# First sort of a two-layer MoE kernel in two parts: one between the scan's later chunks, one beside layer 0

## What is computed

```python
# scan: x, f_logit (2, 5056, 256)
f = lower_bound + (1 - lower_bound) * sigmoid(f_logit)
h[t] = f[t] * h[t-1] + (1 - f[t]) * x[t]
# layer 0 (x = h, 10112 rows)
xn = x / (norm(x) + 1e-6);  en = emb / (norm(emb) + 1e-6)
logits = xn @ en.T / tau
# layer 1 (x = output of layer 0)
logits = x @ w_gate
# both
e = argmax(logits); p = softmax(logits)[e]      # sum + 1e-9
out[row] = p * (relu(x[row] @ w1[e]) @ w2[e])
```

## Time and profile before

| | |
|---|---|
| time, median of 3 runs | 1383.54 us (1382.56 to 1385.02) |
| time of the profiled execution | 1383.36 us |
| its span, first to last instruction | 1381.6 us |
| TensorE busy in the span | 1329.6 us |
| VectorE, ScalarE, GpSimd busy | 971.5, 835.2, 439.2 us |
| mean granted clock | 0.973 |

### The profile page before, as it was taken

One profiled execution on the slowest core, in us unless ns is written; L12 is line 12 of the kernel. 1 busy time (PEld: TensorE's weight loads), 2 busy tenths in 40 slices (PEclk: granted clock), 3 DMA queues, 4 the chain that ended last, 5 costly groups with the idle time before them and its releaser, 6 DMA issues.

```text
span 1381.6 us, 31343 instructions
## 1 busy us (share of the span) xinstructions
PE 1329.6 (96%) x11005; PEld 1299.6 (94%) x11005; DVE 971.5 (70%) x1468; ACT 835.2 (60%) x1402; POOL 439.2 (32%) x458
## 2 busy tenths in 40 slices
PE   7994799999999999999999999999999999999996
PEld 6993399999999999999999999899999999999996
DVE  5878476666666666669876679777777777777773
ACT  4774166666666666666656566556666666666663
POOL 4663221121221211222111234323444444444431
PEclk9995599999999999999999999999999999999999
DMA  8983686666665656668856668546666666666650
GB/s 256 329 275 104 64 273 193 213 199 194 203 198 200 199 195 214 198 193 154 254 166 192 209 202 217 174 153 212 221 217 213 226 226 216 221 213 219 222 186 1
DMA packets 204662, 276.83 MB, mean 200 GB/s; under 512 B 33350, under 2 KB 171988, under 8 KB 204596
## 3 DMA queue, kind: packets, MB, share of 16 engines
q1 hardware_dynamic: 191060, 240.74, 56.7%
q0 software_dynamic: 13536, 35.21, 7.6%
HBM read 242.69 MB, written 35.18 MB: 201 GB/s over the span
## 4 chain that ended last, share of the span: by engine, by line
PE 91%; DVE 4%; issue 1%; ACT 1%; POOL 1%; DMA 1%; SPq 0%; ACTq 0%; DVEq 0%; POOLq 0%
PE bank L1306 39%; PE bank L1324 38%; PE bank L1240 4%; PE bank L1290 3%; PE bank L1335 2%; PE bank L1344 1%; PE bank L1203 1%; PE bank L1222 1%; PE bank L1216 1%; DVE hT L381 1%; DVE gx L371 1%; POOL fg L888 1%; ACT sq L1063 0%; DMA fin<-in_f_logit 0%; ACT th L1049 0%
## 5 line engine op out<-in xcount | busy, mean ns | idle before, releaser
L1306 PE MATMUL bank<-xs,w1h 128*128 128x256 f32 x3008 | 570.5, 288 | 1.5 <-DVE xs L656 1.5
L1119 ACT ACTIVATE hh<-bank 128x512 fp32r<-128x512 f32 x376 | 225.2, 599 | 413.6 <-PE bank L1306 413.6
L1306 PEld LDWEIGHTS bank<-xs,w1h 128*128 128x128 f32 x3008 | 461.5, 189 | 3.2 <-DVE xs L656 1.9
L667 DVE SCALAR_TENSOR_TENSOR hl<-bank,hh 128x512 fp32r<-128x512 f32 x376 | 259.9, 691 | 249.3 <-ACT hh L1119 246.9
L1324 PE MATMUL bank<-w2h,hl 128*128 128x256 f32 x1504 | 423.1, 281 | 0.0
L1324 PE MATMUL bank<-w2l,hh 128*128 128x256 f32 x1504 | 422.5, 281 | 0.0
L1324 PE MATMUL bank<-w2h,hh 128*128 128x256 f32 x1504 | 421.7, 280 | 0.0
L1306 PE MATMUL bank<-xs,w1l 128*128 128x256 f32 x1504 | 421.6, 280 | 0.0
L1306 PEld LDWEIGHTS bank<-xs,w1l 128*128 128x128 f32 x1504 | 283.7, 189 | 0.0
L1324 PEld LDWEIGHTS bank<-w2h,hh 128*128 128x128 f32 x1504 | 283.3, 188 | 0.0
L1324 PEld LDWEIGHTS bank<-w2l,hh 128*128 128x128 f32 x1504 | 283.1, 188 | 0.0
(11 more groups left out here) (160 smaller groups left out, 1039.6 us busy)
## 6 DMA issues: line engine op xcount, KB each, us to landing
w1raw<-in_moe_w SPq DMA_DIRECT2D x94, 1024.0 KB
w2raw<-in_moe_w SPq DMA_DIRECT2D x94, 1024.0 KB, 5.6
rows_b<-yb SPq DMA_DIRECT2D x94, 128.0 KB, 2.3
xin<-in_x SPq DMA_DIRECT2D x19, 512.0 KB, 6.0
fin<-in_f_logit SPq DMA_DIRECT2D x19, 512.0 KB, 7.9
rows_a<-h_rows SPq DMA_DIRECT2D x19, 512.0 KB, 5.6
xb<-rows_a,row_i POOLq DMA_INDIRECT x94, 4.9
xb<-rows_b,row_i POOLq DMA_INDIRECT x94, 4.9
```

Source lines behind the costliest of these rows:

```text
L667: v.scalar_tensor_tensor(hl[:, j, :], bank[j % UB][:, :], 0.0, hh[:, j, :].bitcast(fp32), ALU.max, ALU.subtract).then_inc(hid_lo, 1)
L1119: nc.scalar.activation(hh[:, j, :], bank[j % UB][:, :], ACT.Relu).then_inc(hid_hi, 1)
L1306: ins = mm(bank[j % UB][:, f * GW:(f + 1) * GW], w[:, p, o:o + P], xs[:, p, a, c * GW:(c + 1) * GW], start=k == 0, stop=k == 3 * DC - 1)
```

## The change

- The first sort has two parts, as layer 1's has. `PARTS` lists all four: (0, 40 tiles), (all 79), (0, 64), (all 94). The first part sorts the tokens of chunks 0 to 9 into 12 whole pairs, with 24 slot tiles; the second sorts those left over with the other tokens into 35 pairs, with 70 slot tiles.
- Part 0 runs in ticks between the scan's chunks 11 to 19, three in each, on every engine (`beside_scan`). Part 1 runs in ticks beside layer 0's pairs from pair 0 on. The first 12 pairs gather from the first 5120 rows of `rows_a`.
- SyncE loads the weights of pairs 0 and 1 in those ticks, after it has waited for the experts, and then stores the first pair list (5120 items). The second is stored beside layer 0.
- The chunks from 11 on are written out, not looped.
- Since the second part needs whole chunks in time order, a chunk is loaded with four consecutive tokens on a partition (4 KB in one piece), and the transposes of the load write to PSUM with a step of four, so that time runs along a row as before.
- GpSimd writes its tables of numbers ahead of the scan, and its norms follow the rows by two chunks instead of three.
- Counting takes `EXPERTS_AT_ONCE` = 4, 2, 4, 2 experts with both counts in one PSUM bank.
- In layer 0 the transposes of y stand at one place of a step for both tiles (two steps after the pair), its logits a step later (`old`), each kept with one copy. Layer 1's sorts start later by half a pair and one pair.
- Weights' second buffers share memory with the scan's buffers. VectorE waits for the scan's last stores before the first hidden result.
- For layer 1's second part the waits for the pair list and the stored rows stand behind a gather, beside the wait for the slots.

```diff
+    K1 = 10
+    T1 = K1 * CH
+    P1 = (T1 * P - E * (GW - 1)) // GW
...
+        PARTS = [(0, T1, T1, G * P1, 0, P1), (T1, TT, TT, ST - G * P1, P1, NP - P1),
+                 (0, TA, TA, G * PA, 0, PA), (TA, ST, ST, ST - G * PA, PA, NP - PA)]
+        FRONT = [20, 21, 22, 21]
+        OH_AT = [2, 2, 4, 2]
+        EXPERTS_AT_ONCE = [4, 2, 4, 2]
...
+        def beside(parts):
+
+            def tick(i):
+                if i.var is None and i.const >= NP + 3:
+                    next(parts[3], None)
+                elif i.var is None and i.const >= XA + 3:
+                    next(parts[2], None)
+                elif i.var is None and i.const < XA:
+                    next(parts[1], None)
             return tick
 
-        FRONT = [18, 15]
+        def beside_scan(part):
+            def tick(k):
+                if k.var is None and k.const > K1:
+                    next(part, None)
+            return tick
...
@@ VectorE, scan step
                     v.tensor_tensor_scan(hT[:, c, par, 0:w], fg[:, c, 0:w], gx[:, c, 0:w],
                                          hT[:, c, 1 - par, CW - 1:CW], ALU.mult,
                                          ALU.subtract).then_inc(h_ok, 1)
+                    tick(i)
                 if i.var is not None or i.const > 0:
                     keep_logits(i.plus(-1), CH)
+                tick(i)
...
@@ VectorE, after the scan
+            keep_logits(Index(NCH - 1), tiles_in(NCH - 1))
+            for c in range(DC):
+                split_w1_lo(Index(0), c)
+            finish(parts[0])
+            for half in range(2):
+                split_w2_lo(Index(0), half)
...
@@ SyncE
+            def sort(q):
+
+                lo, hi = PARTS[q][0:2]
+                for _ in range(OH_AT[q] + 2 * len(groups(q)) + 6):
+                    yield
+                if q == 0:
+                    sp.wait_ge(dve_c, mark["experts", q])
+                    for i in (Index(0), Index(1)):
+                        read_expert(i)
+                        load_w1(i)
+                        load_w2(i)
+                        yield
+                sp.wait_ge(dve_c, mark["pair", q])
+                sp.dma_start((rows_av if q < 2 else rows_bv)[:, lo:hi, D:D + 2], pair[:, lo:hi, :]
+                             ).then_inc(pair_out, 16)
...
@@ TensorE
                     for dst, src in ((bank[c], xin), (bank[2 + c], fin)):
+                        in_time = dst[:, 0:nt * P].rearrange("p (q j) -> p q j", j=nt)
                         for j in range(nt):
-                            ins = nc.tensor.transpose(dst[:, j * P:(j + 1) * P],
+                            ins = nc.tensor.transpose(in_time[:, :, j],
                                                       src[:, sx, j * D + c * P:j * D + (c + 1) * P],
                                                       ident[:, :])
...
             def a_step(i):
                 a_front(i, CH if i.var is not None else tiles_in(i.const))
+                tick(i)
+                tick(i)
                 if i.var is not None or i.const > 0:
                     a_back(i.plus(-1), CH)
+                tick(i)
...
+                for b, e, k, number in groups(q):
+                    if b == 0:
+                        pe.wait_ge(dve_c, mark["oh", q])
+                    else:
+                        pe.wait_ge(dve_c, mark["counted", q, b - 1])
+                    mm(sum_of(q, T), ones_b[:, :], oh[:, e:e + k, 0:T], start=True, stop=True)
+                    mm(cum_of(q, T), upto[:, :], oh[:, e:e + k, 0:T], start=True, stop=True).then_inc(pe_s, 1)
+                    yield
+                    yield
...
+            pe.wait_ge(tanh_ok, 2 * NCH)
+            pe.wait_ge(g_ok, 2 * NCH)
+            pe.wait_ge(rows_ok, NCH)
+            pe.wait_ge(lg_kept, NCH)
+            pe.wait_ge(dve_c, mark["slots", 0])
             turn_x(Index(0))
...
@@ TensorE, one pair
                 if here(i) and here(nxt):
                     turn_x(nxt)
+                if here(old) and layer_of(old) == 0:
+                    y_logits(old)
                 if here(last2) and layer_of(last2) == 0:
-                    y_logits(last2, 1)
-                tick(i, 1)
+                    turn_y(last2)
+                tick(i)
...
@@ GpSimd, one pair
+                if i.var is None and i.const == P1 - 3:
+                    pool.wait_ge(dve_c, mark["slots", 1])
+                    pool.wait_ge(pair_out, 32)
+                    for b in range(2):
+                        pool.wait_ge(h_out[b], 16 * ((NCH + 1 - b) // 2))
+                if i.var is None and i.const == NP - 3:
+                    pool.wait_ge(dve_c, mark["slots", 2])
+                if i.var is None and i.const == NP + PA - 3:
+                    pool.wait_ge(dve_c, mark["slots", 3])
+                    pool.wait_ge(pair_out, 64)
                     for s in range(2 * G):
                         pool.wait_ge(y_out[s], stored(s, NP))
```

More of the change, by code:

```diff
@@ L1278, in resort @@
                     yield
-                    if q % 3 == 2:
+                    if q >= 2 and c % 3 == 2:
                         yield
+            parts = [sort(q) for q in range(2 * LY)]
+            tick = beside_scan(parts[0])
+            run_steps(pe, 0, K1 + 1, a_step, LOOP_K, 0)
+            for k in range(K1 + 1, NCH):
+                a_step(Index(k))
+            a_back(Index(NCH - 1), tiles_in(NCH - 1))
+            finish(parts[0])
+            tick = beside(parts)
             def turn_x(i):
```

702 lines of the change are left out of this document (311 added, 391 removed).

## The result

| | before | after |
|---|---|---|
| time, median | 1383.81 us (1382.56 to 1385.02, 20 runs) | 1388.91 us (1383.08 to 1393.68, 20 runs) |
| ratio after / before | | 1.0034, 95% interval 1.0022 to 1.0047 |
| profiled execution, its span | 1383.36, 1381.6 us | 1386.24, 1384.5 us |

The change makes the kernel 5.1 us slower; the forecast was 4.5 us faster. The time lies in the range that was given, the sign is wrong. By the profiled executions the difference is 2.9 us; where the other 2 us are is told with the last of the experiments.

A forecast was written before the change was run, and what follows sets the result against it. TensorE was taken to bound the pairs, one serial sort the gap after the scan. Terms: -42.0 + 22.0 + 21.0 + 0.3 - 5.8 = -4.5 us, forecast 1379.0 us, range 1368 to 1397.

The forecast's parts named there:

- What bounds the kernel: Kernel before: pairs are paid in TensorE time only; between scan and pairs it waits 60.4 us for one serial sort.
- The scan grows: Chunks 11 to 19 carry the first sort: VectorE becomes the bound, a loss of 22 us, bounds 14.4 and 41.
- Rival 3: Scan: lighter TensorE work brings the lower clock for half the stretch; growth 33 in place of 22, 1390 us; chance 0.21.
- The gap: From last scan instruction to first up matmul: shrinks from 60.4 to 18.4 us, a gain of 42.0 us.
- 1.5 us for stores, from 0 to 6: Scan's tail: stores of chunks 16 and 17 land late behind weights and pair list, delaying ScalarE and the last logits.
- slots to first up, 9.3: End of the gap: from slots ready to first up matmul, 10.3 us before, less 1 us for GpSimd, makes 9.3.
- The second sort: Beside layer 0's pairs, where TensorE has no idle time: a loss of 21.0 us, from 18 to 27.
- VectorE's part isn't paid: Second sort: VectorE's 2.2 + 1.5 us per quarter of a pair, against over 5 for TensorE, costs nothing.
- The y path: Layer 0's y transposes and logits in one place, three breaks fewer a pair: a gain of 5.8 us, from 0 to 10.
- Layer 0 at 12.97 us: Sign to look for: a pair of layer 0 takes 12.97 us once the sort is done, not 13.09.
- Edits with no price: 4 KB loads, tables before the scan and weights loaded inside it counted as free; the pair list was excepted, at 1.5 us.
- Rival 2: Scan's transposes: PSUM write with a step of four elements costs like the stepped read, 1395 us; chance 0.12.

The follow-up runs named there:

- the last of the experiments: No new edit: profiled executions of the changed kernel and variants compared over the first chunks; chunk 11's first product comes at 64.7 to 67.1 or 69.5 to 71.0 us.

## Why the prediction was wrong, step by step

- **What bounds the kernel**: right for the kernel before. TensorE has no idle time in its pairs; in the changed kernel it has 3.1 us, in pair 0.
- **The scan grows**: right in size, +22.2 for +22.0. Chunks 11 to 18 take 6.0 to 9.5 us (5.5 to 8 was said), chunks 2 to 10 4.5 to 4.9 (4.5 to 5.0 before). Rival 3 didn't come about in the stated way: the lower level covered 22 us of the stretch in one execution of the changed kernel and 36 in another, and the stretch took 64.1 and 64.8 us. VectorE, not TensorE, is what the chunks wait for.
- **The gap**: mechanism right, size missed by 4.1 us. Slots came at E + 10.7, not E + 9.1: the logits were kept at E + 8.1, where 4.35 and "1.5 us for stores, from 0 to 6" had been counted, and the late store isn't all of it, since without ScalarE's wait they came at E + 5.2 to E + 7.1. The term "slots to first up, 9.3" was 11.8. The 1 us taken off the row of before was right: the second gather's issue ends 5.3 us after the slots, where it was 6.3. What had no term is how long the rows take to land, now that the next weights are issued in front of them: 4.0 us for 1.8.
- **The second sort**: the step that failed, 27.0 us for 21.0. The price of a matmul was right: tables 20.2 forecast, 20.5 where the clock held. Wrong was "VectorE's part isn't paid": it weighed VectorE's busy time per quarter of a pair, where what counts is whether VectorE's result is there when TensorE's queue reaches the matmul. In pair 0 it was not: 3.1 us of wait. The other 2.9 us go with the granted clock, which the sum held at the upper level: it falls twice in the first 20 pairs, for 3.4 us each. A fall costs about 1.7 us: the step from 245.0 us takes 22.73 us, and 20.96 in the kernel with the old y path, which doesn't have it. With the sort a pair later 23.0 are left of the 27.0. This term alone turned the sign: at 27.0 the forecast's own sum gives +1.5 in place of -4.5.
- **The y path**: about -2.8 for -5.8, inside its bounds (the prediction's own 0.12 x 47 is 5.6). The 0.10 us of a plain pair is near the 0.12; the pairs with a sort don't show it. "Layer 0 at 12.97 us" came true at 12.96, and in part for a reason that wasn't mine: 0.03 of the 0.13 is placement.
- **The layers' other terms**: layer 1 was taken as unchanged but for 0.3 us. It fell by 3.3 us, 0.09 for a plain pair, with the same instructions; in the kernel before placement alone did as much and more. No step of the working asked what moving buffers does to TensorE's reads; the edit "weights' second buffers share memory with the scan's" was given no term at all.
- **Edits with no price**: the tables ahead of the scan had the cover "GpSimd idles there". It does, but VectorE doesn't, and the start came 1.5 us later.
- **Rival 2**, the stepped PSUM write, is refuted. The transposes of a load in the changed kernel's scan:

```profile
105.11 0.60 PE L1190 MATMUL bank<-ident,fin 128*128 128x128 f32 x4
```

  0.60 us for four, as with contiguous output. The rule quoted from the Trainium skill's "PSUM — Partial Sum Buffer" doesn't hold for an fp32 transpose with a step of four elements.
- **The choice between cases**: I gave slower a third. The account says that what was counted in busy time was good to 0.4 us, and that what was missed by more was waits between engines, set too low each time, and placement, not set at all. A forecast of -4.5 had no room for that.

The reason under these why the change doesn't pay is in the run with the sort behind the scan. The overlap moves 21 us of VectorE's work beside 34 us of VectorE's work. VectorE had 7.7 us free in 42.2; waits across engines took that back. What is left is a first sort of 40 tiles in place of 79, against a second that has to place all 79 tiles' worth of tokens in TensorE's time.

## What to carry to other kernels

Moving work beside other work pays only with what the engine that does it has free there; ask this of the engine with the longest list, not of the one that waits. Each matmul put into a full TensorE queue needs its operand before its turn, and one that is late stops everything behind it: give it a place by when its producer is done. Look at what is issued to the DMA queues just before a transfer that everything waits for: weights for a later pair can stand in front of it. Before a change to a tuned kernel is timed, hold the addresses of TensorE's operands fixed against each other, or try a gap of 32 bytes; here this was worth more than the change.

## What the runs showed of the hardware that was not expected

- The pace of matmuls (128x256, fp32r) changes with the addresses of TensorE's two operands within a partition. In the kernel before, the start of `xs`, `hh` and `hl` less that of the weights gives 11.94 us a pair of layer 1 at 0 bytes, 11.78 at 544, 11.57 at 576, for the same 96 matmuls. Moving both by 32 bytes, or one by 8 KB, changes nothing there. Three differences give no rule, how large the period is stays open, and the changed kernel's 118.3 ns for 120.0 at equal places says that something else counts, too. The Trainium skill, "TensorE: Matmul & The Clock Gate", Step-by-step: what each phase is for, says that TensorE has two independent read ports and that loading the next weights doesn't steal bandwidth from the running matmul. These runs speak against it as a statement on time: with nothing but addresses changed, the same matmuls take up to 3% longer. That it is these two reads that meet is inferred; no run tells them from the other engines' accesses.
- With a list of 5120 items of 8 bytes and 4 MB of weights on the queues, the slowest 512 KB store took 15.0 to 18.7 us to land in nine executions, where 6.4 was the slowest before; with 2 MB less of the weights 11.4 to 14.2 in three.
- TensorE stayed at its slow pace in the first chunks until 30.8 us in one execution of the kernel with the second sort later, and until 14.3 us in another of the same kernel. The record of the granted clock shows 1.00 in the slow stretch from 17 us on.
